# Filling products of TensorE in the first attention stage: one of 512 columns of zeros in place of three of 128

## The reference

```python
for c in range(nc):                       # 24 chunks of 32 queries
    k_full = concat([mem_k, k[l_start:r_end]]); v_full = concat([mem_v, v[l_start:r_end]])
    scores = scale * q_c @ k_full.T
    scores = scores - max(scores)
    a = exp(scores); a = a / (sum(a) + 1e-9)
    out[c] = a @ v_full
```

## Time and profile before

| | |
|---|---|
| median of three runs | 1165.22 us |
| the profiled execution | 1163.57 us |
| its span | 1161.6 us |
| PE busy | 1145.8 us, 99% of the span |
| DVE, ACT, POOL busy | 926.5, 750.9, 123.3 us |
| mean granted TensorE clock | 0.998 |

### The profile page before, as it was taken

How to read it: one execution, slowest core, us unless ns; L and a number is a source line. 1 busy time by engine, 2 the same in 40 slices (tenths; PEclk the granted TensorE clock), 3 DMA queues, 4 the chain that set the end, 5 groups by cost and what they waited for, 6 DMA issues and landing times.

```text
span 1161.6 us, 20825 instructions
## 1 busy us (share of the span) xinstructions
PE 1145.8 (99%) x7954; PEld 942.8 (81%) x7954; DVE 926.5 (80%) x1419; ACT 750.9 (65%) x1224; POOL 123.3 (11%) x150
## 2 busy tenths in 40 slices
PE   7899999999999999999999999999999999999998
PEld 6788887778888777888888888888888888888887
DVE  5886767776676777777667998988988988988987
ACT  3665555455555555555556877877877877877875
POOL 2052230012233001223100000000000000000000
PEclk9999999999999999999999999999999999999999
DMA  7511412742141374323137100200200200200100
GB/s 261 165 64 55 163 55 95 230 149 91 60 157 55 100 234 158 109 86 105 46 129 264 42 1 1 73 1 1 72 0 0 72 0 0 72 0 0 37 1 37
DMA packets 40720, 94.05 MB, mean 81 GB/s; under 512 B 4288, under 2 KB 4288, under 8 KB 40640
## 3 DMA queue, kind: packets, MB, share of 16 engines
q1 hardware_dynamic: 40640, 92.95, 23.7%
HBM read 80.35 MB, written 12.58 MB: 80 GB/s over the span
## 4 chain that ended last, share of the span: by engine, by line
PE 94%; DVE 3%; issue 1%; DMA 1%; ACT 0%; SPq 0%; POOL 0%; ACTq 0%; POOLq 0%; DVEq 0%
PE ps_h L1253 9%; PE ps_h L1255 9%; PE ps_h L1260 9%; PE ps_h L1417 7%; PE ps_h L1412 7%; PE ps_h L1413 7%; PE ps_y L1456 7%; PE ps_y L1452 7%; PE ps_y L1450 7%; PE ps_y L1332 5%; PE ps_y L1337 5%; PE ps_y L1333 4%; PE ps_h L1235 2%; PE ps_h L1211 2%; PE ps_y L1321 1%
## 5 line engine op out<-in xcount | busy, mean ns | idle before, releaser
L1253 PE MATMUL ps_h<-xop,wop 128*128 128x512 f32 x484 | 188.3, 389 | 0.0
L1255 PE MATMUL ps_h<-xop,wop 128*128 128x512 f32 x484 | 188.3, 389 | 0.0
L1412 PE MATMUL ps_h<-x_split,weights 128*128 128x512 f32 x384 | 149.4, 389 | 0.0
L1413 PE MATMUL ps_h<-x_split,weights 128*128 128x512 f32 x384 | 149.4, 389 | 0.0
L1260 PE MATMUL ps_h<-xop,wop 128*128 128x512 f32 x484 | 149.0, 389 | 0.0
L1450 PE MATMUL ps_y<-weights,hid 128*128 128x512 f32 x360 | 140.0, 389 | 0.0
L1452 PE MATMUL ps_y<-weights,hid 128*128 128x512 f32 x360 | 140.0, 389 | 0.0
L878 DVE TENSOR_TENSOR wop<-rawp,wop 128x448 fp32r<-128x448 f32 x144 | 91.1, 661 | 32.7 <-ACT wop L494 32.7
L757 ACT ACTIVATE tmp<-ps_h 128x512 f32<-128x512 f32 x96 | 57.2, 595 | 92.4 <-PE ps_h L1417 92.4
L899 DVE TENSOR_TENSOR x_raw<-ps_h,probs_t 128x512 f32<-128x512 f32 x70 | 48.1, 687 | 79.6 <-PE ps_h L1260 79.3
L1332 PE MATMUL ps_y<-hid,wout 128*128 128x512 f32 x264 | 105.7, 400 | 0.6 <-DVE stage_h L930 0.3
(11 more groups left out here) (103 smaller groups left out, 2277.9 us busy)
## 6 DMA issues: line engine op xcount, KB each, us to landing
rawp<-wgv_l SPq DMA_DIRECT2D x36, 512.0 KB, 3.8
oraw<-wo_l SPq DMA_DIRECT2D x72, 256.0 KB, 3.9
unit<-v_l SPq DMA_DIRECT2D x24, 512.0 KB, 4.5
unit<-k_l SPq DMA_DIRECT2D x24, 368.0 KB, 4.2
unit<-q_l SPq DMA_DIRECT2D x24, 256.0 KB, 3.4
x_stage<-y_dram SPq DMA_DIRECT2D x6, 1024.0 KB, 5.7
out<-stage SPq DMA_DIRECT2D x24, 256.0 KB, 2.3
braw<-wb_l SPq DMA_DIRECT2D x11, 512.0 KB, 5.6
```

Of the source, the lines that this page charges most:

```text
L1253: nc.tensor.matmul(dst, w_h[k], xop[:, m, 0, k, :], start=first and k == 0, stop=False, skip_group_check=True)
L1255: nc.tensor.matmul(dst, w_l[k], xop[:, m, 0, k, :], start=False, stop=False, skip_group_check=True)
L1412: nc.tensor.matmul(dst, lhs(c, 0), x_split[:, 0, c, :], start=(c == 0), stop=False)
L1413: nc.tensor.matmul(dst, lhs(c, 1), x_split[:, 0, c, :], start=False, stop=False)
```

## The change

At the filling places of the first stage one product of the identity with 128x512 zeros replaces the three products of 128 columns. A float32 product is two weight loads and two MATMULs, so four TensorE instructions stand in place of twelve. The first place of the kernel keeps its six narrow products (`WARM` is now 6 and used there alone). Place (0, 0), which held one narrow product, is left empty, and place (0, 1), which held one, now holds a wide one. The zeros are written by GpSimd in a new memset behind the identity, in memory that the hidden features of the dense layer take later; PE waits for it (`ident_done` at 3) ahead of the first wide product.

```diff
-WARM = 3
+WARM = 6
@@ build
+        zeros = at("zeros", 155648, [P, 512])
@@ gpsimd
+            nc.gpsimd.memset(zeros[:], 0.0).then_inc(ident_done, 1)
@@ tensor
+            def wide_fill():
+
+                nc.tensor.matmul(ps_y[:, 3, :], ident[:], zeros[:], start=True, stop=True)
+
@@ attention
                     scores(a)
                     if b == 1:
-                        warm_up(WARM)
+                        pe.wait_ge(ident_done, 3)
+                        wide_fill()
                         scores(b)
@@ fill_first
                 elif (p, place) == (4, 1):
-                    warm_up(WARM)
+                    wide_fill()
                     early_product(1, M2)
-                elif place != 2:
-                    warm_up(1 if p == 0 and place < 2 else WARM)
+                elif place != 2 and (p, place) != (0, 0):
+                    wide_fill()
 
             pe.wait_ge(ident_done, 2)
-            warm_up(2 * WARM)
+            warm_up(WARM)
```

## The result

The changed kernel is slower. Sixteen runs of it took 1163.73 to 1172.30 us, median 1168.90; sixteen of the kernel before, in rounds with it, 1163.02 to 1167.10, median 1165.23. The ratio is 1.0029, 95% interval 1.0019 to 1.0038: +3.4 us, with +2.2 to +4.4 as its ends (the two medians lie 3.7 apart). The forecast was 1164.4 in a range up to 1167.0: the sign was wrong, and the time lies outside the range.

The account below looks back on a forecast made before the run. PE was taken to wait for its own instructions, 256 at a time. -0.1 to -1.6 at `scores(7)`, -0.36, and +0.1 to +0.5 for fills were taken as -0.8: 1165.22 to 1164.4 us, range 1160.8 to 1167.0.

Parts of the forecast that it names:

- PE waits for its own instructions, in blocks of 256: First stage: waits by "issue" of 0.60 to 1.38 us stand at block boundaries; one of about 1.1 us goes before scores(6) ends.
- A wide fill is 0.20 longer, and ACT's steps and the waits for instructions cover it: First-stage fills: 0.87 against 0.67 us; 0.00 to 0.10 a fill kept, 0 to 1.4 over fourteen, mostly swallowed by waits.
- The load of k holds `scores(2)` at 14.5: Unit 2, first stage: the 1.07 wait goes, but k lands only at 14.4, so scores(2) starts at 14.5, not 14.71.
- The walk along the blocks: First stage to unit 6: blocks about 5.3 us after v's issue, at 18.5, 24.0, 29.55, 35.35; 37.5 against 38.5, -1.0.
- From there to the end of the stage: -0.1 to -1.6, then no more waits: After unit 6: scores(7) ends between 41.9 and 43.4 against 43.49; behind it PE works through, without 0.36 of waiting.
- From 61.20 on the time is carried to the end one for one: Behind the first stage: whatever its chain ends earlier or later than 61.20 passes unchanged to the kernel's end.
- The columns decide: Rival, first-stage fills: uncovered at 0.2 us each, waits as many and as long; +2.8, time 1168.0; chance 0.10.
- The fetch gets out of the way of the loads: Rival, first stage: blocks asked for before v's load, so the waits vanish; -4.2, time 1161.0; chance 0.24.
- The clock: Rival, first stage: PE staying at 2.4 GHz gives -0.3 to -0.8 more; another slow stretch up to +1.4; chance 0.10.

Follow-up runs that it names:

- three_172: The kernel before with each filling product 172 columns of zeros instead of 128 of the identity, still twelve instructions a fill; 1165.38 us, ratio 0.9997.
- wide_v_late: The changed kernel with first-stage v of unit g+2 asked for when scores(g+2) is done, about 2 us later; 1165.44 us, ratio 0.9991 to before.
- wide_v_late_124: The changed kernel with later v loads and 31 tiny products (124 instructions) at the first stage's end; 1162.54 us, once more 1163.23; ratios to before 0.9978, 0.9984.
- wide_plus_124: The changed kernel with 31 tiny float32 products (124 TensorE instructions) behind the last wide fill of the first stage; 1167.50 us, ratio 1.0019 to before.
- one_384: The changed kernel with 384 instead of 512 columns in its one product, still four instructions a fill; 1169.56 us, ratio 1.0039 to before.
- narrow_plus_132: The kernel before with 33 tiny float32 products (132 TensorE instructions) at the end of its first stage; 1166.54 us, ratio 1.0008.
- no_fills: The changed kernel without its sixteen wide products, the six narrow ones at the start kept; 1170.85 us, ratio 1.0042 to before.

## Why the prediction was wrong, by its own steps

- *PE waits for its own instructions, in blocks of 256.* Right, and the count placed the four boundaries from `weigh_values(2)` to (5) to the record. The Trainium skill ("Runtime: NRT & Kernel Launch", "Instruction fetch mechanics") has crossing a boundary mostly hidden; this stage again disagrees, with 1.06 to 1.58 us at each of them.
- *A wide fill is 0.20 longer, and ACT's steps and the waits for instructions cover it.* Right on the whole: 0.86 against 0.67, and three_172 shows that the length costs nothing that can be measured. ACT's steps cover less than was kept, though: from the start of a fill to what follows it took 0.95 beside the copy and 1.05 beside `stage_x`, where 0.89 and 0.87 were before, 0.24 a unit; the waits for instructions took it up.
- *The load of k holds `scores(2)` at 14.5.* Right: 14.73.
- *The walk along the blocks.* Right up to unit 6: blocks were forecast at 18.5, 24.0, 29.55 and 35.35; the last three came at 24.05, 29.71 and 35.69. DVE took up unit 6 at 38.23, where 37.5 was forecast and 38.58 was before: of the gain of 1.0 us, 0.35 was left, since each block was a little later (0.34 by the last) and the fill and scores behind it took 1.84 where 1.6 was put.
- *From there to the end of the stage: -0.1 to -1.6, then no more waits.* This step failed. The walk's own rule, a block 5.3 us behind the issue of v, was dropped one unit too soon. Carried on, it gives the block of `weigh_values(5)` at 41.2 and the end of `scores(7)` at about 43.6; the sum took 41.9 to 43.4, whose lower half doesn't even follow from its own 1 to 1.8 us of wait in place of 0.76 (with 37.5 and the 5.0 us from `scores(6)` to `scores(7)` before, that is 42.7 to 43.5). Measured were 1.58 us of wait and 43.55 + 0.86 = 44.41. The next boundary, in `weigh_values(6)`, was never counted out and stood in the sum at nothing, as "PE works through"; it cost 1.40. The one wait saved ahead of `scores(6)` only went behind it.
- *From 61.20 on the time is carried to the end one for one.* This failed too. Behind the first stage every instruction of PE stands 124 places earlier in its blocks, and two more attention stages and the loads near 620 us depend on that. In the first trace it cost 3.6 us, in the second 0.8. wide_v_late against wide_v_late_124, which differ only in the tiny products, and the changed kernel against wide_plus_124 give 0.8 to 2.9 us, all of one sign, each within overlapping intervals; the forecast had no term for it.
- *The rivals.* "The columns decide" gave nearly the right time (1168.0), by luck and by the wrong mechanism: one_384 has fewer columns and is as slow. "The fetch gets out of the way of the loads" is real, and was bought with an edit of the loads, not by this change. The clock kept its upper level through the first stage in the first trace of the changed kernel (granted 1.00); in the second it was 0.83 on average between 40 and 50 us, and the stage ended only 0.46 later. A stretch at the lower level, which the kernel before has too, is not what makes the difference.

The measured parts: +2.5 us in the first stage (two traces: 2.52, 2.95) instead of -0.8, and the rest of the +3.4 to +4 behind it. The first number stands against one trace of before; against narrow_plus_132, whose first stage is the same, it would be +4.1 and +4.5, so the division between the stage and what follows is known to 1.5 us at best. What stays open is how the second part divides: the waits of the third stage and near 620 us vary between traces by more than their mean. Also open is at which instruction a block is asked for. In the changed kernel and the one before, packets started 1.4 to 3.9 us behind the boundary before them, and only the part due to the v load was tested. The first stages of wide_v_late and of the two runs with tiny products (-0.90, -1.73 and -1.93) differ by less than narrow_plus_132 does from before.

## What to carry to other kernels

Where a stage consists of many small products, count TensorE's instructions as a resource with its own deliveries: 256 at a time, two per MATMUL with its load and four per float32 product, and look in the timeline for runs of equal records that are cut by a wait with no semaphore (a wait by "issue" at the head of a run can be one for another engine, as in no_fills). Taking instructions out moves every later boundary of the program; a saving of 124 instructions cost 3.4 us here, and putting 124 useless ones back at a harmless place, with one load asked for 2 us later, turned it into a gain of 2.3 to 2.8 (the second of these just within its interval). So add up the waits at all boundaries on both sides of the change, to the end of the stage and in every later stage of small products, before the sum is closed.

## What the runs showed of the hardware that was not expected

- The fetch of a block of instructions goes with the traffic of the loads. Ahead of the waits that end at 19.16 and 25.17 in the kernel before, and of all five in the changed one, the packet starts 2.7 to 3.2 us after the issue of a v load of 512 KB. With the later v loads it starts ahead of that issue or within 0.7 us of it, and the waits are half. It is not the whole of it: at 33.63 to 43.04 in the kernel before the packets start ahead of v's issue or within 1.2 us of it, and PE still waits 0.76 to 1.18. PE goes on 2.2 to 2.8 us after the packet's start.
- The order of a fetch and a load can tip between two executions of the same instructions: waits of 1.38 and 0.60 us in the trace of before, none in that of narrow_plus_132.
- The granted clock falls to its lower level for over 40 us when the fills go (0.50 between 10 and 50 us), although PE is busy 76% of the time by its records.
- The spread of single executions is wider than three runs suggest: 1163.7 to 1172.3 us for the changed kernel, against 1165.1 to 1166.0 in the three runs of before that stood at the start.
